# Pooled attention, soft mixture of experts and a squared-ReLU layer: logits and slot inputs are formed from the attention weights, without the attention's result x

## What is computed

```python
# 1. attention on pooled keys and values
k_p = k.reshape(B, H, 72, 8, 64).mean(axis=3)
v_p = v.reshape(B, H, 72, 8, 64).mean(axis=3)
scores = (1 / 8) * np.matmul(q, k_p.transpose(0, 1, 3, 2))
attn = np.exp(scores - scores.max(-1, keepdims=True)); attn /= attn.sum(-1, keepdims=True) + 1e-09
x = np.matmul(attn, v_p)                 # then reshaped to (4608, 512): the heads side by side
# 2. soft mixture of 8 experts with 4 slots each
logits = x @ phi                         # (4608, 32)
d = np.exp(logits - logits.max(0)); d /= d.sum(0) + 1e-09
slot_input = (d.T @ x).reshape(8, 4, 512)
slot_out[e] = np.maximum(slot_input[e] @ w1[e], 0) @ w2[e]
c = np.exp(logits - logits.max(1)); c /= c.sum(1) + 1e-09
y = c @ slot_out
# 3. the last layer
r = np.maximum(y @ w_in, 0.0)
out = (s * (r * r) + b) @ w_out
```

## Time and profile before

| | |
|---|---|
| median of three executions | 719.61 us (718.86 to 720.09) |
| the profiled execution: its own time | 722.03 us |
| its span, first to last instruction | 720.2 us |
| share of the chain that ended last: PE, DVE, DMA, issue, POOL | 77%, 12%, 4%, 3%, 2% |
| mean granted TensorE clock | 0.965 |

### The profile page before, as it was taken

The page is one execution under the profiler, slowest core; times in us unless marked ns, Lnnn a source line. Parts: engine busy times, 40 slices in busy tenths (PEclk is TensorE's granted clock), DMA queues, the critical chain, the costliest instruction groups (busy, mean ns, idle before and its releaser), DMA issues.

```text
span 720.2 us, 10697 instructions
## 1 busy us (share of the span) xinstructions
PE 674.5 (94%) x3929; PEld 545.3 (76%) x3929; DVE 435.7 (60%) x673; ACT 335.8 (47%) x598; POOL 114.6 (16%) x132
## 2 busy tenths in 40 slices
PE   4379999999998989999999999999999999999997
PEld 2368988888987323788888888888888888888885
DVE  6788898895774472866545445454454554544543
ACT  1236776766762123655444444444444444444442
POOL 1565775673231000000000000000000000000000
PEclk8568999999999989999999999999999999999999
DMA  7987779668368996000001001000010000100101
GB/s 199 213 199 207 214 201 225 202 164 344 118 239 302 388 430 277 1 1 30 30 1 58 1 1 59 0 30 29 0 58 0 26 32 0 58 1 0 59 1 58
DMA packets 31368, 80.29 MB, mean 111 GB/s; under 512 B 6497, under 2 KB 14689, under 8 KB 28513
## 3 DMA queue, kind: packets, MB, share of 16 engines
q1 hardware_dynamic: 31328, 79.76, 34.5%
HBM read 70.32 MB, written 9.44 MB: 111 GB/s over the span
## 4 chain that ended last, share of the span: by engine, by line
PE 77%; DVE 12%; DMA 4%; issue 3%; POOL 2%; ACT 1%; ACTq 0%; DVEq 0%
PE bank L1281 18%; PE bank L1282 18%; PE bank L1283 18%; PE bank L1145 5%; PE bank L1265 4%; DVE kp L771 4%; DMA kvbuf<-in_v_dram 3%; PE bank L1128 3%; PE bank L1236 2%; PE bank L1109 2%; PE bank L1215 2%; DVE ex L830 2%; DVE mx L818 1%; PE bank L1055 1%; POOL ex L575 1%
## 5 line engine op out<-in xcount | busy, mean ns | idle before, releaser
L975 DVE SCALAR_TENSOR_TENSOR win_sb<-win_sb,sb_col 128x512 f32<-128x512 f32 x144 | 108.5, 753 | 197.7 <-ACT win_sb L714 197.6
L1281 PE MATMUL bank<-w_hi,r_hi 128*128 128x512 f32 x576 | 224.2, 389 | 1.4 <-DVE r_lo L981 1.4
L1282 PE MATMUL bank<-w_lo,r_hi 128*128 128x512 f32 x576 | 224.1, 389 | 0.0
L1283 PE MATMUL bank<-w_hi,r_lo 128*128 128x512 f32 x576 | 224.1, 389 | 0.0
L714 ACT ACTIVATE win_sb<-bank 128x512 f32<-128x512 f32 x144 | 86.1, 598 | 217.8 <-PE bank L1265 217.8
L1281 PEld LDWEIGHTS bank<-w_hi,r_hi 128*128 128x128 f32 x576 | 108.1, 188 | 24.4 <-DVE r_lo L981 2.0
L1283 PEld LDWEIGHTS bank<-w_hi,r_lo 128*128 128x128 f32 x576 | 108.2, 188 | 22.4
L1282 PEld LDWEIGHTS bank<-w_lo,r_hi 128*128 128x128 f32 x576 | 108.1, 188 | 22.4
L981 DVE SCALAR_TENSOR_TENSOR r_lo<-win_sb,sb_col,r_hi 128x512 fp32r<-128x512 f32 x144 | 107.5, 747 | 1.5 <-ACT r_hi L723 1.5
L723 ACT ACTIVATE r_hi<-win_sb,sb_col 128x512 fp32r<-128x512 f32 x144 | 103.2, 717 | 1.6 <-PE bank L1283 1.6
L1145 PE MATMUL bank<-vx,aT 72*128 72x96 f32 (+1 forms) x640 | 70.5, 274 | 5.2 <-issue 4.6
(11 more groups left out here) (130 smaller groups left out, 528.6 us busy)
## 6 DMA issues: line engine op xcount, KB each, us to landing
late<-in_moe_w_dram SPq DMA_DIRECT2D x8, 2048.0 KB, 16.3
kvbuf<-in_k_dram SPq DMA_DIRECT2D x16, 576.0 KB
kvbuf<-in_v_dram SPq DMA_DIRECT2D x16, 576.0 KB
out_dram<-win_sb SPq DMA_DIRECT2D x36, 256.0 KB, 2.4
qbuf<-in_q_dram SPq DMA_DIRECT2D x8, 1024.0 KB, 11.8
early<-in_moe_w_dram SPq DMA_DIRECT2D x4, 2048.0 KB, 11.8
early_third<-in_moe_w_dram SPq DMA_DIRECT2D x2, 2048.0 KB, 11.7
win_sb<-in_moe_w_in_dram SPq DMA_DIRECT2D x4, 1024.0 KB, 6.2
```

The source lines that it names most:

```text
L975: dve.scalar_tensor_tensor(out=g_sb[:, n % 2, :], in0=r_sb[:, n % 2, :], scalar=sb_col[:, 0:1], in1=r_sb[:, n % 2, :], op0=ALU.mult, op1=A ...
L1281: pe.matmul(acc, r2_hi[:, f % 2, toks], w_hi[:, f, :], start=(f == 0), stop=False)
L1282: pe.matmul(acc, r2_hi[:, f % 2, toks], w_lo[:, f, :], start=False, stop=False)
L1283: last = pe.matmul(acc, r2_lo[:, f % 2, toks], w_hi[:, f, :], start=False, stop=(f == F2C - 1))
```

## The change

1. **No x.** The pooled values times phi (`vphi`, 72 x 32 for each head) are kept apart from the values. The logits are formed from the turned weights alone: the stationary operand is the 32 columns of one head's `vphi`, the moving one the weights of 256 tokens, and four heads (or head pairs) use the four column quarters of the array; a product with `fold` adds the quarters and turns the result.
2. **Slot inputs.** `d` is multiplied with the attention weights `ex` (kept for 12 units), which gives 32 x 72 for each head (`b_sb`, L1265, L1267); that is turned (`bT`, L1280) and multiplied with the pooled values in natural order (`vn`, L1294). A running maximum and a running sum (`tops`, `falls`, `sums`) stand where partial sums were. The group is now one batch with half of the mixed tile: 8 groups in place of 5.
3. **Token pairs of one head are turned.** A unit is now two tiles of one batch and four heads (again 36 units). The transposition takes two neighbouring tokens of one head straight from `qbuf`; the gathering copy is gone. Both halves of `k_bd` hold the same head, so `k_bd` is twice as large.
4. **Keys and values on 128 partitions.** A piece is three of the nine groups of 8 tokens that one of 128 (batch, head, eighth) rows has, 6 KB in one run; the ring has three pieces. Each pooled piece is written twice, so that one transposition gives both halves. VectorE pools two of three key pieces, GpSimd the third and the values.
5. **Buffers.** The first five weight matrices are loaded during the attention, not three. The products that kept TensorE at work near the end of the attention (`KEEP_WARM`, L1084) are gone.

The core of the diff:

```diff
-    KEEP_WARM = {TILES + 2: 1, TILES + 3: 1, TILES + 6: 1, TILES + 8: 2}
+    EARLY = 5
+    EXR = 12
+        def group_step(g):
+            return TPP * (g // 2) + (MIXED if g % 2 == 0 else TPP - 1) + 5
+        STEPS = group_step(B - 1) + 6
+        MAX_AT, EXP_AT, B_AT, BT_AT, SUMS_AT = 1, 2, (2, 3), 4, 5
...
 @block.sync
-        kv_v = [t.rearrange("b h (g r) d -> g b h (r d)", r=POOL) for t in (k, v)]
+            rows = (k, v)[which][2 * i:2 * i + 2].rearrange("b h (x g r) d -> (b h x) g (r d)", x=GH, r=POOL)
...
 @block.gpsimd
+                for copy in range(2):
+                    pool.tensor_tensor((kp, vp)[which][:, GP * u:GP * (u + 1), copy, :], buf[:, :, 0:HD], buf[:, :, HD:2 * HD],
+                                       ALU.add).then_inc((k_pooled_pool, v_pooled)[which], 1)
...
 @block.scalar
-                act.activation(q_tile[:, t % 2], qbuf[j // QT][:, :, j % QT, :], ACT.Copy).then_inc(q_gathered, 1)
-                    act.activation(x_of[i % 2][:, t % TPP, :].rearrange("p (a g) -> p a g", a=HP),
+                    act.activation(l4[:, l4_cols(U)], bank[L_B][:, 0:P if is_mixed(U) else L4], ACT.Copy).then_inc(l4_kept, 1)
...
 @block.vector
-                dve.tensor_reduce(logits[:, t, :], head_logits(x_banks[:, :], HP, XP, "s a t"),
+                for g in groups_at(n, MAX_AT):
+                    dve.wait_ge(pmT_ready, g + 1)
+                    dve.reduce_max(tops[:, 0, g:g + 1], bank[MISC][:, 0:P], AX.X).then_inc(misc_read, 1)
+                for i, u, g in dve_keys(n):
+                    pool_keys(i, u, g)
+                if n == 1:
+                    pool_values(1)
...
 @block.tensor
-                        last = pe.transpose(bank[Q_B][:, P * a:P * (a + 1)], q_tile[:, t % 2, 2 * a:2 * a + 2, :].rearrange("p h d -> p (h d)"), ident[:, :])
+                            src = qbuf[w][:, HB * unit_half(U) + a, j0:j0 + 2, :].rearrange("p j d -> p (j d)")
+                for g in groups_at(n, MAX_AT):
+                    pe.wait_ge(pm_ready, g + 1)
+                    misc_free("top", g)
+                    for quad in range(QUADS):
+                        last = pe.matmul(bank[MISC][QUAD * quad:QUAD * (quad + 1), 0:P], pm[:, :], ident[:, :], start=True, stop=True)
-                                last = pe.matmul(bank[X_B[g]][toks, col:col + VC],
-                                                 aT[:, t % 2, h, toks], vx_of[i % 3][:, (H * bb + h) // 2, VC * (h % 2):VC * (h % 2 + 1)],
+                            last = pe.matmul(bank[L_B][QUAD * a:QUAD * (a + 1), 0:L4], vphi[:, H * bb + HB * unit_half(U) + a, :],
+                                             aT[:, U % 2, 2 * a:2 * a + 2, :].rearrange("k j p -> k (j p)"),
+                for g in groups_at(n, SUMS_AT):
+                    misc_free("sums", g)
+                for g in groups_at(n, MAX_AT):
+                    pe.wait_ge(top_ready, g + 1)
+                    misc_free("row", g)
```

More of the change, by code:

```diff
@@ new lines, in values_pooled @@
+        def values_pooled(i, u):
+            if values_by_dve(i, u):
+                return v_pooled_dve, 2
+            return v_pooled, 2 * sum(not values_by_dve(ii, b) for ii in range(i + 1) for b in range(PIECES if ii < i else u + 1))
+        MISC_USES = sorted([(U + 5, 1, "logits", sum(closes_logits(o) for o in range(U + 1))) for U in range(UNITS) if closes_logits(U)] +
+                           [(group_step(g) + MAX_AT, 0, "top", g) for g in range(B)] +
+                           [(group_step(g) + MAX_AT, 3, "row", g) for g in range(B)] +
+                           [(group_step(g) + SUMS_AT, 2, "sums", g) for g in range(B)])
@@ new lines, in query_bank_free, with turn_pooled @@
+            def query_bank_free(n):
+                keys, values, weights, naturals = first_query_bank(n)
+                for i, u in keys:
+                    pe.wait_ge(kT_kept, 2 * (PIECES * i + u + 1))
+                for i, u in values:
+                    pe.wait_ge(vT_kept, 2 * (PIECES * i + u + 1))
+                for i in weights:
+                    pe.wait_ge(wv_kept, i + 1)
+                for i, half in naturals:
+                    pe.wait_ge(vn_kept, 2 * i + half + 1)
+            def turn_pooled(pooled, out, u):
+                for a in range(GP):
+                    twice = pooled[:, GP * u + a].rearrange("p c d -> p (c d)")
+                    last = pe.transpose(out[:, P * a:P * (a + 1)], twice, ident[:, :])
+                return last
@@ L1190, in _ @@
-            for c in range(DC):
-                last = pe.matmul(bank[6][:, SLOTS * c:SLOTS * (c + 1)], slot_cols[:, P * c:P * (c + 1)], fold[:, 0, :],
-                                 start=(c == 0), stop=True, skip_group_check=True)
-            last.then_inc(sT_psum, 1)
-            pe.wait_ge(dsum_ready, 2 * GROUPS)
-            pe.matmul(small_bank(GROUPS - 1)[:, 200:201], dsum.rearrange("p a s -> p (a s)"), ones[:, :],
-                      start=True, stop=True).then_inc(den_ready, 1)
+                U = n - 4
@@ new lines, in _ @@
+                U = n - 5
+                if 0 <= U < UNITS and closes_logits(U):
+                    e = logits_closed(U)
+                    pe.wait_ge(fold_ready, 2)
+                    pe.wait_ge(l4_kept, e + 1)
+                    misc_free("logits", e + 1)
+                    for j in range(1 if is_mixed(U) else 2):
+                        last = pe.matmul(bank[MISC][:, SLOTS * j:SLOTS * (j + 1)], l4[:, l4_cols(U)][:, P * j:P * (j + 1)], fold[:, 0, :],
+                                         start=True, stop=True)
+                    last.then_inc(lg_ready, 1)
@@ L1198, in turn_c @@
+                for g in groups_at(n, MAX_AT):
+                    pe.wait_ge(top_ready, g + 1)
+                    misc_free("row", g)
+                    pe.matmul(bank[MISC][:, 0:SLOTS], tops[0:SLOTS, 1, g:g + 1].to_broadcast([SLOTS, P]), ident[0:SLOTS, 0:SLOTS],
+                              start=True, stop=True).then_inc(row_ready, 1)
             def turn_c(n):
```

1071 lines of the change are left out of this document (553 added, 518 removed).

## The result

The changed kernel takes 737.2 us (median of 4 runs, 734.17 to 740.24), the kernel before 719.24 us on the same chip (4 runs, 716.95 to 720.09). The ratio is 1.0255, interval 1.0205 to 1.0305: 2.5% slower. The forecast was 706.

The account below looks back on a forecast made before the run. TensorE was taken to bound the unchanged last 486.2 us and the steps, loads the start. Start -15.4, steps -6.0, tail +6.0, slot stage +1.8 make -13.6: 722.0 to 708.4, median 2.4 lower, 706 us; own range 698 to 716.

Parts of the forecast that it names:

- The start: Loads of queries, keys and values up to the first turned weights: expected at 34 us, 15.4 earlier.
- The test named in the prediction: Sign for the start: DMA above 350 GB/s in the first 20 us.
- the first piece of pair 1's keys decides: At the start, VectorE's list has this load next, so its landing at 24.4 us sets the first turned weights.
- The price of the new products: TensorE's own work in the attention steps, summed from prices per instruction: 42.0 us a pair of batches.
- a sign of being wrong: In the attention steps, narrow products above 60 ns would show the forecast wrong.
- Rival 4: Narrow products in the steps do not overlap: 14 us more a pair, 762 us in all; chance 0.08.
- The waits in front of bank 7: TensorE waits for VectorE in two of nine steps, 1.3 and 1.7 us, making 45.0 to 45.4 a pair.
- The clock: Granted clock taken as 1.00 in the pair windows; half clock adds up to 3 us in the tail.
- rival 2: The clock falls at the waits of the eight groups in the steps: +14, 720 us; chance 0.12.
- The tail: Last group's slot inputs, one engine after another: 16.4 us against 10.4, +6.0, bounds 14 and 19.
- w1 came cold: At the start of the slot stage TensorE comes to w1 at the low clock: +1.8 us.
- The sum: Whole kernel: start, steps, tail and slot stage together -13.6 us, giving 706 us.

Follow-up runs that it names:

- e6: Changed kernel with VectorE pooling the last piece of pair 0's values ahead of the first piece of pair 1's keys: 737.83 us.
- e7: Changed kernel with e1, e2 and e6 together, and the running maximum taking its second operand as a scalar: 707.44 us.
- e11: Changed kernel plus throwaway identity products ahead of the last group's waits in the tail only: 737.13 us.
- e1: Changed kernel with VectorE's reduction of the turned maxima, running maximum and fall moved to the head of their step: 721.6 us.
- e2: Changed kernel with each group's slot sums written to bank 6 instead of bank 7: 727.5 us.
- e3: Changed kernel plus four identity products ahead of the slot sums' wait and four ahead of the row's wait: 725.6 us.
- e9: Changed kernel plus the same added products as e3, each set one place later, behind the sums and behind the row: 735.97 us.

## Why the prediction was wrong

*The start* was right. First turned weights 34 us predicted, 33.6 measured. The DMA engines moved 279 GB/s up to there, where the earlier trace rows has 200. The test named in the prediction, above 350 in the first 20 us, was missed, as this window shows (last number):

```profile
0.00:20.00 20.00, 10.89 (x31) 5.81 (x32) 10.92 (x13) 5.27 (x9) 10.47 (x17) 0.96 0.95 332
```

No run undid the new loads; that they are the cause is read from the traces, not tested. That the first piece of pair 1's keys decides holds in part: VectorE waited 1.2 us for it, at 24.45 us as forecast (24.4), but without it in the way (e6) the start was only 0.9 us earlier. And the 221 GB/s of the earlier trace rows, which the prediction took as agreeing with the Trainium skill's figure for partitions 0 to 63, belong to loads on 72 partitions; no row here tests that figure.

*The price of the new products* was right in the sum, 1.0 us a pair too low. 42.0 us a pair was predicted; e7, at a clock of 1.00, has TensorE busy for 43.05 in its pair. Single prices were off both ways: sixteen instructions of L1280 were put at 64 ns and took 65, L1239's at 58 and took 71 (above the 60 ns that was named as a sign of being wrong), the shortest at 46 and took 22. Rival 4 (products that do not overlap, 762) is out.

*The waits in front of bank 7* were too small. The prediction had 3.0 to 3.4 us a pair, which over four pairs is 14 at most; the trace has 16.2, and in its pair window TensorE stands still for 6.8. It saw that VectorE reads `top` behind maximum, sum and difference, but it put the comparison at a small operation. Seven of them took 0.92 us on average, because they start beside GpSimd's normalisation. And where slot sums and row fall in one step, it charged 1.7 us; TensorE paid 0.90 and then 1.75 us.

*The clock* is the step that failed. The sum was made with the clock at 1.00 in the steps, as the two pair windows of the earlier trace rows had it, and charged the low clock only to the tail (up to 3) and to w1 (1.8). The changed kernel was granted 0.90 from the first turned weights to w1. With two levels, 1.2 and 2.4 GHz, a mean of 0.90 over 215.7 us is 43 us at the low one, and half of that, up to 21.6 us, is what it cost. The same stretch of e7 has 0.97 over 186.6 us, up to 5.6.

The busy and idle time of the two stretches divide the 29.1 us between them. TensorE is busy for 184.6 us in the changed kernel and for 169.8 in e7 with the same work: 14.8 us, which the lower clock accounts for (the means allow up to 16.0). It stands still for 31.2 and 16.9: 14.3 us are waits. In the pair, 45.0 to 45.4 us became 54.6: 1.0 from the products, 4.8 from the clock, which the prediction had at nothing there, and 3.4 to 3.8 from waits that it had too short.

This is rival 2, which had a chance of 0.12 and +14 us. Its mechanism was right; it priced one fall of 1.7 us a group. In the steps a fall outlasts the products right behind the wait: 3.63 us at the low level and part of the next 4.19, all of it on work that TensorE then waits for nobody to do. With waits longer than forecast beside it, the time went past the 720 of rival 2, to 737.

*The tail* was 18.5 us (from the last logits at 230.8) against 16.4 predicted, inside its bounds of 14 to 19, and mostly at the low level (0.54 behind the row); filling it gave 3.1 back (e11), where the prediction had up to 3; w1 came cold and cost 2.3 more than before against 1.8.

*The sum.* Start -15.8 measured against -15.4. To w1's first product 249.3 against 218.6 predicted: 30.7 us, nearly all of the 31.2 between 737.2 and 706. e7, which removes the waits and computes the same, reaches w1's first product at 218.6 and takes 707.4. The estimate described a kernel that does not wait, and this one does. That e7 hits it is partly luck: its start is 2 us better and its products 1 us a pair dearer.

*What stays open*: why some waits are followed by a fall and others are not (in the changed kernel 0.77 us alone was, and pairs of 2.1 to 2.7 us in one step were; 0.81 at 71.92 and 1.76 at 60.48 were not), and how much of e1's and e2's gain is wait and how much clock, since each takes away both.

## What to carry to other kernels

Where one engine is busy throughout, a wait put into its stream costs itself and what the clock loses behind it: price the two together, and look at the granted clock of the stretch before and after before taking new work at the old price. When several small results share a PSUM bank, the order in which the reading engine takes them decides whether the writing engine stops; moving one 0.24 us reduction, with the two small operations behind it, to the head of its step was worth 15.6 us here. If waits remain, throwaway products ahead of them can be worth more than they cost (11.6 us in e3), and one place later they gained almost nothing (e9); taking the waits away is worth more (e7).

## What the runs showed of the hardware that was not expected

- Two idle stretches of 0.90 and 1.75 us within 3.37 us, in a stream that was otherwise busy at a clock of 1.00, were followed by 3.63 us at the low level with TensorE busy all the time; eight score instructions took 2.13 us instead of 1.15.
- A VectorE `tensor_tensor` of 128x1 took 1.05 us beside a GpSimd instruction that had begun 0.11 us before it, and 0.16 us elsewhere; as a `tensor_scalar` it took 0.21 beside the same instruction.
- Sixteen instructions (eight products) with 72-row weights and 64 columns streamed, in quarters of the array, started 22 ns apart (L1293 in e7), half of the cheapest price in the earlier trace rows.
